# Two score tiles taking turns on VectorE in a top-k attention loop, with both masks made in the next step

## The reference, cut to what matters

```python
def attention(q, k, v):              # 4 batches, 8 heads, 576 rows, head size 64
    scores = matmul(q, k.T) / sqrt(64)
    kth = partition(scores, -32)[..., -32]        # the 32nd largest score of each row
    scores = where(scores >= kth, scores, -1e9)
    attn = exp(scores - max(scores))
    return matmul(attn / (sum(attn) + 1e-9), v)   # becomes x [2304, 512]

def dense(x, w_in, w_out):           # w_in [512, 2048], w_out [2048, 512]
    h = x @ w_in
    return (h * cos(h)) @ w_out

def experts(x, ...):                 # 8 experts, each token goes to one
    e = argmax(x @ w_gate)
    return gate[e] * sigmoid_gate[e] * (relu(x @ w1[e]) @ w2[e])
```

## Time and profile before

| | us |
|---|---|
| median of 3 runs (lowest, highest) | 1443.74 (1442.76, 1446.47) |
| the profiled execution's own time | 1439.62 |
| its span | 1438.0 |
| TensorE busy | 1275.0 (89%) |
| VectorE busy | 933.8 (65%) |
| ScalarE busy | 655.6 (46%) |
| GpSimd busy | 560.5 (39%) |

### The profile page before, as it was taken

The page is one execution under the profiler, slowest core; times in us unless marked ns, Lnnn a source line. Parts: engine busy times, 40 slices in busy tenths (PEclk is TensorE's granted clock), DMA queues, the critical chain, the costliest instruction groups (busy, mean ns, idle before and its releaser), DMA issues. The chain is left out here.

```text
span 1438.0 us, 18220 instructions
## 1 busy us (share of the span) xinstructions
PE 1275.0 (89%) x5962; PEld 805.4 (56%) x5963; DVE 933.8 (65%) x1690; ACT 655.6 (46%) x1082; POOL 560.5 (39%) x696
## 2 busy tenths in 40 slices
PE   4557899999999999899899998899599999999996
PEld 2435656857647658567567576584244444444443
DVE  6999998899999999999899999533111111111110
ACT  3455665766666766766757666542011111111110
POOL 2444562464554654554554645515211111111110
PEclk9768999999999999999999999999799999999998
DMA  8201001101001100100010000003313433251000
GB/s 247 88 8 24 1 8 36 37 8 39 9 16 33 32 16 8 25 23 18 17 47 1 1 15 1 8 8 132 136 59 119 149 141 141 80 181 49 14 13 1
DMA packets 81839, 71.52 MB, mean 50 GB/s; under 512 B 62266, under 2 KB 62266, under 8 KB 81248
## 3 DMA queue, kind: packets, MB, share of 16 engines
q1 hardware_dynamic: 76192, 60.86, 13.2%
q0 software_dynamic: 5568, 9.65, 2.1%
HBM read 62.97 MB, written 11.45 MB: 52 GB/s over the span
## 5 line engine op out<-in xcount | busy, mean ns | idle before, releaser
L720 DVE MAX8 tops<-scores_left 128x8 f32<-128x576 f32 x432 | 327.2, 758 | 12.3
L407 POOL TENSOR_TENSOR probs<-scores,probs 128x576 f32<-128x576 f32 x144 | 212.3, 1474 | 241.5 <-ACT probs L514 241.5
L976 PE MATMUL dense_banks<-x_T,weights 128*128 128x256 f32 x1024 | 249.4, 399 | 17.0 <-ACT h_T L552 17.0
L864 DVE COPY x_gathered_T<-score_banks 128x512 f32<-128x512 f32 x25 | 17.3, 691 | 347.6 <-PE score_banks L1100 347.6
L986 PE MATMUL dense_banks<-weights,h_T 128*128 128x512 f32 x512 | 236.4, 605 | 0.0
L976 PEld LDWEIGHTS dense_banks<-x_T,weights 128*128 128x128 f32 x1024 | 198.4, 199 | 59.6 <-ACT h_T L552 21.1
L723 DVE MATCH_REPLACE8 scores_left<-tops,scores_left 128x576 f32<-128x576 f32 x288 | 213.8, 742 | 0.0
L1126 PE MATMUL dense_banks<-weights,expert_h_T 128*128 x400 | 178.2, 598 | 17.4 <-DVE expert_h_T L869 17.3
L1110 PE MATMUL score_banks<-weights,x_gathered_T 128*128 x400 | 178.5, 600 | 1.1 <-DVE x_gathered_T L864 1.1
L514 ACT ACTIVATE probs<-scores,top_consts 128x576 f32<-128x576 f32 x144 | 111.5, 775 | 122.3 <-POOL top_consts L404 122.0
L986 PEld LDWEIGHTS dense_banks<-weights,h_T 128*128 128x128 f32 x512 | 93.5, 193 | 107.0 <-issue 107.0
(11 more groups left out here) (160 smaller groups left out, 1544.9 us busy)
## 6 DMA issues: line engine op xcount, KB each, us to landing
weights<-in_moe_w SPq DMA_DIRECT2D x16, 2048.0 KB, 10.9
y_rows<-y_rows_sb SPq DMA_DIRECT2D x18, 256.0 KB, 2.0
k_rows<-in_k SPq DMA_DIRECT2D x32, 128.0 KB, 2.7
q_rows<-in_q SPq DMA_DIRECT2D x16, 256.0 KB, 3.5
v_rows<-in_v SPq DMA_DIRECT2D x32, 128.0 KB, 2.4
weights<-in_moe_w_in SPq DMA_DIRECT2D x1, 4096.0 KB, 13.0
weights<-in_moe_w_out SPq DMA_DIRECT2D x1, 4096.0 KB, 22.5
k_rows<-in_k SPq DMA_DIRECT2D x16, 32.0 KB, 2.6
```

Of the source, the lines that this page charges most:

```text
L407: nc.gpsimd.tensor_tensor(ex, SS[:, u % 3, i, :], ex, ALU.subtract).then_inc(s["masked_done"], 1)
L720: V.max(top, src).then_inc(s["tops_done"], 1)
L976: last = MM(HO[:, f % 2, 0:BT], win[:, kd, f * P:(f + 1) * P], XT[:, m % 2, kd, :], start=kd == 0, stop=kd == KD - 1)
```

## The change

The work rows become two, one for each tile. `top_k` becomes `top_op(u, i, op)`, one of a tile's seven operations, and the loop goes over the operations outside and the tiles inside: MAX8 of tile 0, MAX8 of tile 1, MATCH_REPLACE8 of tile 0, and so on. Each operation still waits for the one before it of its own tile, which is now the last but one on the engine. `tops_at` gives the count of `tops_done` at which an operation is done. The reciprocals stand behind operation 5 (the third MATCH_REPLACE8) of tile 0. `reduce_h` is split: its first instruction stands behind operation 2 of both tiles, its second behind operation 3.

On GpSimd both masks of step `st - 2` now stand at the head of the iteration, one after the other, and the second `gate` ahead of the denominators. On ScalarE both `below` stand ahead of `copy_scores`, and both `exps` behind it and the second half of the sine.

```diff
@@ helper
+def tops_at(u, i, op):
+    return 14 * u + 2 * op + i + 1
@@ tiles
-        WK = sb("scores_left", [P, S], stack=att)
+        WK = sb("scores_left", [P, 2, S], stack=att)
@@ GpSimd, mask
-                pool.wait_ge(s["tops_done"], (2 * u + i) * 7 + 7)
+                pool.wait_ge(s["tops_done"], tops_at(u, i, 6))
@@ GpSimd, loop
                 if 0 <= u < NS:
+                    mask(u, 0)
                     mask(u, 1)
                 gate(st, 0)
+                gate(st, 1)
                 if 0 <= u < NS:
                     pool.wait_ge(s["exps_done"], 2 * u + 2)
...
-                gate(st, 1)
-                if 0 <= st - 1 < NS:
-                    mask(st - 1, 0)
                 gate(st, 2)
@@ ScalarE, loop
                 if 0 <= st - 2 < NS:
+                    below(st - 2, 0)
                     below(st - 2, 1)
                 if st < NS:
                     copy_scores(st)
...
                 if 0 <= st - 2 < NS:
+                    exps(st - 2, 0)
                     exps(st - 2, 1)
                 for m, i in dense:
                     if i < 4:
                         copy_h(m, 4 * i)
                         copy_h(m, 4 * i + 1)
-                if 0 <= st - 1 < NS:
-                    below(st - 1, 0)
                 if 0 <= u < NS:
                     copy_probs(u)
-                if 0 <= st - 1 < NS:
-                    exps(st - 1, 0)
@@ VectorE
-            def top_k(u, i):
...
+            def top_op(u, i, op):
+                rnd = op // 2
+                top = TOP[:, u % 3, i, rnd * 8:rnd * 8 + 8]
+                src = SS[:, u % 3, i, :] if op < 2 else WK[:, i, :]
+                if op == 0:
+                    if i == 0:
+                        dve.wait_ge(s["scores_copied"], u + 1)
+                    at_least(dve, s["consts_done"], 2 * (u - 3) + i + 1)
+                else:
+                    dve.wait_ge(s["tops_done"], tops_at(u, i, op - 1))
+                if op % 2 == 0:
+                    V.max(top, src).then_inc(s["tops_done"], 1)
+                else:
+                    V.match_replace(WK[:, i, :], top, src, NEG).then_inc(s["tops_done"], 1)
...
             for st in range(LOOP):
-                if 0 <= st - 1 < NS:
-                    top_k(st - 1, 0)
-                for m, i in block_at(st):
-                    if i in (2, 4):
-                        reduce_h(m, (i - 2) // 2)
-                if 0 <= st - 1 < NS:
-                    top_k(st - 1, 1)
-                elif st - 2 == NS - 1:
-                    reciprocals(NS - 1)
+                for op in range(7):
+                    for i in range(2):
+                        if 0 <= st - 1 < NS:
+                            top_op(st - 1, i, op)
+                        if op == 5 and i == 0 and 0 <= st - 2 < NS:
+                            reciprocals(st - 2)
+                    for m, i in block_at(st):
+                        if i in (2, 4) and op in (2, 3):
+                            reduce_h(m, (i - 2) // 2, op - 2)
```

More of the change, by code:

```diff
@@ L708, in _ @@
             V = nc.vector
-            def top_k(u, i):
[L711 to L719, removed]
-                    V.max(top, src).then_inc(s["tops_done"], 1)
[L721 to L725, removed]
+            def top_op(u, i, op):
[9 more added lines that the diff above has]
+                if op % 2 == 0:
+                    V.max(top, src).then_inc(s["tops_done"], 1)
+                else:
+                    V.match_replace(WK[:, i, :], top, src, NEG).then_inc(s["tops_done"], 1)
             def reciprocals(u):
@@ L730, in reciprocals, with reduce_h @@
                 V.reciprocal(RD[:, u % 2, :], DEN2[:, u % 2, :]).then_inc(s["rden_done"], 1)
-            def reduce_h(m, g):
-                dve.wait_ge(s["dense_emptied"], m * MOE_FILLS + 8 * (g + 1))
-                at_least(dve, s["gated_done"], (2 * (m - 1) + g + 1) * 4)
+            def reduce_h(m, g, part):
                 hs = HS[:, g * 8:(g + 1) * 8, :].rearrange("p a n -> p (a n)")
                 r1 = R[:, g, :, :].rearrange("p a n -> p (a n)")
[L737 to L740, removed]
-            for st in range(LOOP):
-                if 0 <= st - 1 < NS:
-                    top_k(st - 1, 0)
-                for m, i in block_at(st):
-                    if i in (2, 4):
-                        reduce_h(m, (i - 2) // 2)
-                if 0 <= st - 1 < NS:
-                    top_k(st - 1, 1)
-                elif st - 2 == NS - 1:
-                    reciprocals(NS - 1)
+                if part == 0:
+                    dve.wait_ge(s["dense_emptied"], m * MOE_FILLS + 8 * (g + 1))
+                    at_least(dve, s["gated_done"], (2 * (m - 1) + g + 1) * 4)
+                    V.tensor_scalar(r1.bitcast(I32), hs, 1.0 / TWO_PI, None, ALU.mult).then_inc(s["reduced_done"], 1)
+                else:
+                    dve.wait_ge(s["reduced_done"], m * 4 + 2 * g + 1)
+                    V.scalar_tensor_tensor(out=r1, in0=r1.bitcast(I32), scalar=-TWO_PI, in1=hs,
+                                           op0=ALU.mult, op1=ALU.add).then_inc(s["reduced_done"], 1)
+            for st in range(LOOP):
+                for op in range(7):
[7 more added lines that the diff above has]
+                            reduce_h(m, (i - 2) // 2, op - 2)
             chain = [0]
```

## The result

| | us |
|---|---|
| after, median of 4 runs (lowest, highest) | 1502.76 (1500.62, 1509.25) |
| before, median of 4 runs | 1443.25 |
| ratio, 95% interval | 1.0419, 1.038 to 1.0457 |
| the profiled execution after, its span | 1502.42, 1500.8 |

The account below looks back on a forecast made before the run. VectorE was taken to bound the attention loop, with TensorE close behind. 115 - 26 - 16 = 73 us off the profiled 1439.62 gives 1366.6, carried to 1368 us for the median; range 1343 to 1408.

Parts of the forecast that it names:

- Part 1: VectorE's top search: two tiles taking turns overlap operations, a step 9.95 us instead of 11.55, 115 us less over 72 steps.
- lower bound of 65 us: VectorE's search: gain left of 115 us if a value load starts only when the engine is empty.
- Part 3: Both masks at the next step's head: covered in plain steps, VectorE stalls 1.6 us in 16 sine steps, 26 us given back.
- 1.7 us to spare: Plain step: margin by which the denominators (6.0 us) precede VectorE's reciprocals (7.75 us).
- Part 4: TensorE becomes as long as VectorE, 88 to 91 us a block against 90.5; 2 us a block stay, 16 us given back.
- about 3.5 us: How late TensorE can be before the copy of scores, and with it the reciprocals, are late too.
- (a): Rival: value loads cost more, or TensorE's products wait for copies of h behind two exponentials; 1390 to 1420 us, chance 0.22.
- (d): Slower rival: no overlap on VectorE and the mask chain's delays in full at 16 sine steps; 1452 to 1464 us, chance 0.07.
- 26 + 16 us: Loss terms: 26 us of VectorE stalls at sine steps, 16 us from TensorE being level but not in step with VectorE.

Follow-up runs that it names:

- masks-alone run: Changed kernel with VectorE's list as before (one tile after the other, one work row), both masks still at the head of the next step: 1499.73 us, 1.0382.
- constants-first run: Changed kernel with GpSimd making the constants of both tiles before the first subtraction: 1399.95 us, 0.969.
- fastest version: Changed kernel with both tiles' constants made before the first subtraction and ScalarE's first two copies of h moved ahead of the exponentials: 1362.35 us, 0.9461.
- offset version: Changed kernel with operations 0 to 3 of a tile alternating with 4 to 6 of the tile before, one mask at the head, one mid-iteration: 1427.17 us, 0.9913.

## Why the prediction was wrong

*Part 1 was right.* Forecast 9.95 us of work a step, measured 9.8; a value load behind a replace that it doesn't wait for overlaps like the rest, 0.66 us from start to start, so the lower bound of 65 us wasn't needed. On the page "VectorE: DVE Perf Modes", section "The DRAIN you can't avoid", the Trainium skill has the next operation wait for an empty pipe and a semaphore cost nothing extra; it also says that a next operation which isn't held starts earlier, which the prediction left out. For MAX8 and MATCH_REPLACE8 these runs bear out that second statement, and a wait is not free: 0.795 us with a wait on the operation in front and 0.66 without.

*Part 3 was wrong, and with it the sign.* The step that failed is its timetable: "From the last MAX8 at 0: the first compare runs until 0.4". It started the masks when their tops are ready. ScalarE isn't free then: its list holds the copy of x first, which waits for TensorE's products with the values, and the masks begin behind it (489.71 and 492.34 above, with constants ready since 486.6; 4.2 us late in the median step). I saw the two GpSimd round trips and checked them against VectorE's reciprocals, with 1.7 us to spare; the instruction that they delayed was the copy of scores behind the second compare, and TensorE behind it. The diff showed that order, and the front part says that the transposes wait for that copy. The masks-alone run puts the price of this part at 53 us (1499.7 against 1446.5) without any gain on VectorE, and the constants-first run shows that the second compare's wait behind the first subtraction carries more than all of it. The stalls of VectorE that this part did price, 1.6 us in 16 places and 26 us in all, were 176 us in 56 places between 100 and 880 us, and cost nothing of their own.

*Part 4 held in its own terms.* TensorE's 88 to 91 us a block is the bound where the loop is short: in the fastest version it is 97.6% busy, nothing comes of moving VectorE's reciprocals, and its quietest blocks take 90.9 us, though others take 92 to 105. That version's last MAX8 starts at 845.49 us and its time is 1362 us, close to the 845 and 1368 that were forecast for the changed kernel; this speaks for Parts 1 and 4 and does nothing for Part 3, and that it comes so close is in part luck, since its blocks and stalls are not those of the sum. Its slack of "about 3.5 us" rested on the timetable of Part 3.

*The rivals.* (a) named the copies of h behind two exponentials, 16 places with 2 to 3 us. The wait at place 3 is there, 3.04 us, but it took moving them to see that they are worth 70 us in this kernel. None of my slower rivals had overlap and still lost: (d) asked for "No overlap", and the measured slowdown came with full overlap. The missing rival was a loop over three engines that doesn't contain the one that got faster.

*Small readings.* The earlier trace rows names "issue" as what the four reciprocals waited for, not another engine, and the earlier trace rows shows 15 of each reduction in its stretch, 16 being the count of the whole loop. Neither bears on the sum.

*The sum.* 115 us fewer on VectorE came to nothing here (masks alone, with and without turns: 1500 and 1502 us). What I called given back, 26 + 16 us, was a loop that by itself takes 53 us more than the kernel before.

*Idle time and clock.* The sum had no term for the clock, and some of the loss is there. The same 5962 products are busy 1299.8 us in the changed kernel and 1264.9 us in the constants-first version, whose clock between 200 and 800 us is 0.99 where the changed kernel's is 0.95. So of the 104 us between the two profiled executions (1502.42 and 1398.41) about 35 are products that took less time and about 69 are time in which TensorE idled. Before the change the products took 1275.0 us, so by the same reckoning about 25 of the 63 us lost are slower products. This is an estimate from modelled ends of products, not an experiment.

Left open: the masks-alone run also moves the second `gate` and the exponentials, which were not tried by themselves, and the offset version was not mended.

## What to carry to other kernels

When work is moved in one engine's list, note for each engine what it does last before the moved piece, and start the timetable there and not where the data are ready. Then follow every copy behind the moved piece to who waits for it. In-order lists close loops over several engines; a faster engine outside the loop is worth nothing (0 us here), and the same speed-up is worth 36 us when the loop is opened, so look for the loop first: waits on all engines while none is full. Two round trips to another engine should be issued together, both requests ahead of the first answer's use; here the order of four small instructions was worth 102 us.

## What the runs showed of the hardware

GpSimd's two-input subtraction, 1.41 us alone, took 3.39 us where it ran beside VectorE's two-input reduction of h, which took 2.28 us. The timeline of both in the changed kernel:

```profile
510.05 2.28 DVE L742 SCALAR_TENSOR_TENSOR reduced_h<-reduced_h,h_T 128x2048 f32<-128x2048 int32 x1
```

```profile
510.21 3.39 POOL L412 TENSOR_TENSOR probs<-scores,probs 128x576 f32<-128x576 f32 x1 [5.18 <-ACT probs L518]
```

It is longer by 2.0 us, about as long as the two overlapped (2.1 us), in the middle of the loop. It can't explain much of the slowdown: all 144 subtractions together take 219.1 us in the changed kernel and 212.3 in the one before.
